# Matmuls of queries with state and scores with values issued one at a time between projection matmuls, instead of in blocks of six

## The reference

```
q, k, v, f_logit: (B=4, H=8, S=768, D=48)
f = sigmoid(f_logit)
for t in range(S):
    state = f[t] * state + k[t] outer v[t]      # 48 x 48 per batch and head
    y[t]  = q[t] @ state
x = y as rows: 3072 tokens x 384
xn = x / rms(x) * rms_g
x  = (silu(xn @ w_gate) * (xn @ w_val)) @ w_out  # d_ff 1536
h  = x @ w_in                                    # d_ff 2048
g  = 0 below -1, h above 1, (h + 1)**2 / 4 between
out = g @ w_out2
```

## Time and profile before

| | |
|---|---|
| median of 3 runs | 1015.99 us |
| span of the profiled execution, first to last instruction | 1013.9 us |
| TensorE matmuls | 1000.9 us busy, 99% |
| TensorE weight loads | 985.1 us busy, 97% |
| DVE | 586.5 us, 58% |
| ACT | 342.7 us, 34% |
| POOL | 19.5 us, 2% |
| mean granted TensorE clock | 0.999 of full speed |
| L334, queries with state | 192 instructions, 278 ns mean |
| L338, scores with values | 384 instructions, 265 ns mean |

### The profile page before, as it was taken

How to read it: one execution, slowest core, us unless ns; L and a number is a source line. 1 busy time by engine, 2 the same in 40 slices (tenths; PEclk the granted TensorE clock), 3 DMA queues, 4 the chain that set the end, 5 groups by cost and what they waited for, 6 DMA issues and landing times.

```text
span 1013.9 us, 16822 instructions
## 1 busy us (share of the span) xinstructions
PE 1000.9 (99%) x6307; PEld 985.1 (97%) x6307; DVE 586.5 (58%) x1196; ACT 342.7 (34%) x624; POOL 19.5 (2%) x58
## 2 busy tenths in 40 slices
PE   7999999999999999999999999999999999999998
PEld 7899999999999999999999999999999999999998
DVE  8777564665565664664663665545554545454553
ACT  2343322322322322222222444344344443434343
POOL 0000000000000000000000000000000000000000
PEclk9999999999999999999999999999999999999999
DMA  5541111111111011111121230000000000000000
GB/s 187 185 143 40 40 39 41 39 39 47 31 46 39 31 47 39 39 39 39 39 68 48 80 92 2 1 23 0 23 0 23 0 23 0 23 0 23 0 24 24
DMA packets 15768, 42.22 MB, mean 42 GB/s; under 512 B 1408, under 2 KB 8064, under 8 KB 15744
## 3 DMA queue, kind: packets, MB, share of 16 engines
q1 hardware_dynamic: 15744, 41.88, 12.3%
HBM read 37.16 MB, written 4.72 MB: 41 GB/s over the span
## 4 chain that ended last, share of the span: by engine, by line
PE 93%; DVE 4%; issue 1%; POOL 1%; ACT 0%; DMA 0%; POOLq 0%; DVEq 0%
PE gate_ps L399 14%; PE val_ps L399 14%; PE acc L475 13%; PE gate_ps L463 10%; PE val_ps L463 10%; PE acc L421 9%; PE acc L479 7%; PE acc L425 5%; PE y_ps L338 4%; PE tb L313 2%; PE y_ps L334 2%; PE tb L322 2%; DVE qd L717 1%; PE ta L299 1%; DVE kd L726 1%
## 5 line engine op out<-in xcount | busy, mean ns | idle before, releaser
L833 DVE TENSOR_TENSOR h_lo<-h_buf,h_hi 128x384 fp32r<-128x384 f32 x224 | 123.2, 550 | 13.2 <-ACT h_hi L644 6.2
L475 PE MATMUL acc<-h_hi,w_hi 128*128 128x384 f32 x381 | 127.5, 335 | 0.0
L475 PE MATMUL acc<-h_hi,w_lo 128*128 128x384 f32 x381 | 127.3, 334 | 0.0
L637 ACT ACTIVATE act_buf<-act_buf,half_col 128x384 f32<-128x384 f32 x128 | 78.7, 615 | 140.4 <-DVE act_buf L883 140.4
L580 ACT ACTIVATE act_buf<-gate_ps 128x384 f32<-128x384 f32 x96 | 47.2, 491 | 180.9 <-PE gate_ps L399 180.9
L399 PE MATMUL gate_ps<-x_hi,w_hi 128*128 (+1 forms) x288 | 100.5, 349 | 2.0 <-DVE h_buf L822 1.5
L585 ACT ACTIVATE h_hi<-h_buf 128x384 fp32r<-128x384 f32 x96 | 50.4, 525 | 151.0 <-DVE h_buf L828 151.0
L421 PE MATMUL acc<-h_hi,w_hi 128*128 128x384 f32 x288 | 100.4, 349 | 0.0
L399 PE MATMUL val_ps<-x_hi,w_hi 128*128 (+1 forms) x288 | 100.2, 348 | 0.0
L399 PE MATMUL gate_ps<-x_hi,w_lo 128*128 (+1 forms) x288 | 96.7, 336 | 0.0
L421 PE MATMUL acc<-h_hi,w_lo 128*128 128x384 f32 x288 | 96.6, 335 | 0.0
(11 more groups left out here) (117 smaller groups left out, 2040.5 us busy)
## 6 DMA issues: line engine op xcount, KB each, us to landing
raw<-qkf_dram SPq DMA_DIRECT2D x21, 768.0 KB, 4.3
x<-wb_dram SPq DMA_DIRECT2D x12, 576.0 KB, 5.9
v_sb<-v_dram SPq DMA_DIRECT2D x24, 192.0 KB, 2.8
out_dram<-x SPq DMA_DIRECT2D x7, 576.0 KB, 2.8
raw<-wc_dram SPq DMA_DIRECT2D x7, 384.0 KB, 3.1
x<-qkf_dram SPq DMA_DIRECT2D x2, 768.0 KB, 6.5
kd<-wc_dram SPq DMA_DIRECT2D x3, 384.0 KB, 3.2
qd<-wc_dram SPq DMA_DIRECT2D x3, 384.0 KB, 3.4
```

The costliest lines, as they stand in the source:

```text
L475: pe.matmul(acc[:, m, 0:N], wc_part(w, j, 1, m), h_hi[:, j % 2, :], start=(j == 0 and w is w_hi), stop=False)
L637: nc.scalar.activation(act_buf[:, j % 2, :], act_buf[:, j % 2, :], ACT.Square, bias=half_col[:, :], scale=0.5).then_inc(square_ready, 1)
L833: nc.vector.tensor_tensor(h_lo[:, j % 2, :], h_buf[:, j % 2, :], h_hi[:, j % 2, :].bitcast(F32), ALU.subtract).then_inc(done, 1)
```

## The change

attend is called with a single step (0 to 5) instead of issuing its six matmuls. A new function, between, issues step m behind the m-th matmul of the nine of the projection group that follows the slot: behind each of the first six matmuls of value 3, project_out 2, project_out 5, gate 7, gate 10 and value 10. The semaphore waits of the block stand at its first step, y_made's increment at its last. turn_kd and turn_x also take an index, but are still called in full at their slots, and first_attention keeps its order. The number of instructions is the same on every engine, and nothing changes on ACT, DVE, POOL and SP.

```diff
...
-                def attend(n, c, half):
-                    if half == 0:
+                def attend(n, c, half, step):
+                    p, part = half * NP // 2 + step // 3, step % 3
+                    o = p * 2 * D
+                    if half == 0 and step == 0:
                         pe.wait_ge(scores_ready, n * 2 + 2)
                         pe.wait_ge(decayed_ready, n + 1)
                         if not isinstance(n, int) or n > 0:
                             pe.wait_ge(xs_ready, n)
-                    for p in range(half * NP // 2, (half + 1) * NP // 2):
-                        o = p * 2 * D
-                        pe.matmul(y_ps[:, o:o + 2 * D], qd[0:PR, c % 2, p, :], decayed[0:PR, p, :],
-                                  start=True, stop=False, skip_group_check=True)
-                        for r in range(2):
-                            h = slice(o + r * D, o + (r + 1) * D)
-                            mm = pe.matmul(y_ps[:, h], scores[:, r, p, :], v_sb[:, r, p, :],
-                                           start=False, stop=True, skip_group_check=True)
-                    mm.then_inc(y_made, 1)
-
...
                         elif o == 8:
                             update(n)
-                        elif o == 9:
-                            attend(n, c, 0)
-                        elif o == 10:
-                            attend(n, c, 1)
                         elif o == 13:
-                            turn_x(n)
+                            for k in range(KM):
+                                turn_x(n, k)
+
+                def between(i, slot, m):
+
+                    if i is None or m > 5:
+                        return
+                    for c in range(CT):
+                        n = i * CT + c
+                        o = slot - WINDOW * c
+                        if o == 9 or o == 10:
+                            attend(n, c, o - 9, m)
 
...
-                def project(i, j, part, bank):
+                def project(i, j, part, bank, following, slot):
 
                     par = i % 2
                     for k in range(KM):
-                        for w, x in ((w_hi, x_hi), (w_hi, x_lo), (w_lo, x_hi)):
+                        for t, (w, x) in enumerate(((w_hi, x_hi), (w_hi, x_lo), (w_lo, x_hi))):
                             mm = pe.matmul(bank[:, 0:N], wb_part(w, j, part, k), x[:, par, k, :],
                                            start=(k == 0 and x is x_hi and w is w_hi),
                                            stop=(k == KM - 1 and w is w_lo))
+                            if k < KM - 1 or t < 2:
+                                between(following, slot, 3 * k + t)
                     return mm
 
-                def gate(i, j):
+                def gate(i, j, following=None, slot=0):
                     pe.wait_ge(w_lo_ready, j + 1)
                     if j == 0:
                         pe.wait_ge(x_lo_ready, i * CT + CT)
                     pe.wait_ge(gate_used, i * JB + j + 1)
-                    project(i, j, 0, gate_ps).then_inc(gate_made, 1)
-
-                def value(i, j):
+                    project(i, j, 0, gate_ps, following, slot).then_inc(gate_made, 1)
+
+                def value(i, j, following, slot):
                     pe.wait_ge(h_ready, i * JB + j + 1)
-                    project(i, j, 1, val_ps).then_inc(val_made, 1)
-
-                def project_out(i, j):
+                    project(i, j, 1, val_ps, following, slot).then_inc(val_made, 1)
+
+                def project_out(i, j, following=None, slot=0):
                     pe.wait_ge(h_hi_ready, i * JB + j + 1)
                     if j == 0:
                         pe.wait_ge(x2_ready, i + 1)
                     for m in range(KM):
-                        for w in (w_hi, w_lo):
+                        for t, w in enumerate((w_hi, w_lo)):
                             pe.matmul(acc[:, m, 0:N], wb_part(w, j, 2, m), h_hi[:, j % 2, :],
                                       start=(j == 0 and w is w_hi), stop=False)
+                            between(following, slot, 2 * m + t)
                     pe.wait_ge(h_lo_ready, i * JB + j + 1)
                     for m in range(KM):
                         mm = pe.matmul(acc[:, m, 0:N], wb_part(w_hi, j, 2, m), h_lo[:, j % 2, :],
                                        start=False, stop=(j == JB - 1))
+                        if m < KM - 1:
+                            between(following, slot, 2 * KM + m)
                     mm.then_inc(out_made, 1)
 
                 def gated_mlp(i, following):
 
                     for j in range(JB):
                         if j > 0:
-                            gate(i, j)
+                            gate(i, j, following, 3 * j - 1)
                         if following is not None:
                             attention(following, 3 * j)
-                        value(i, j)
+                        value(i, j, following, 3 * j)
                         if following is not None:
                             attention(following, 3 * j + 1)
                         if j > 0:
-                            project_out(i, j - 1)
+                            project_out(i, j - 1, following, 3 * j + 1)
                         if following is None and j == 0:
                             pe.wait_ge(least_ready, NCH + 1)
                             pe.transpose(ta[0:1, 0:P], least[:, NP:NP + 1], ident[:, :]).then_inc(least_turned, 1)
```

## The result

The kernel with single steps took 1026.78 us (median of 4 runs, 1026.56 to 1026.95) against 1015.97 for the kernel before: ratio 1.0105, 95% interval 1.0093 to 1.0117. It is 10.8 us slower. The forecast was 1028.2 us.

The account below looks back on a forecast made before the run. TensorE, busy 99% of the span, was taken as the bound. Steps +0.8, late y_made +7.3 in second and +4.1 in first chunks, third 0, sum to +12.2 us over the median of 1015.99: 1028.2 us, range 1016 to 1035.

Parts of the forecast that it names:

- Part 1, the steps themselves: On TensorE, six single steps cost 1.39 us against 1.37 for a block; over 42 blocks +0.8 us.
- 12 bare loads: Lower bound for the steps on TensorE: only 12 loads per block, 1.34 us, giving -1.3 us in all.
- the 0.03 of leftover per block: Block's 1.37 us beyond its 12 loads on TensorE; paid at every step it gave the upper bound, +6.5 us.
- Part 2, second chunk: y_made 1.04 us later passes whole through ACT, POOL and DVE to gate 8's load: 7 x 1.04 = +7.3 us.
- Part 2, first chunk: Late y_made, less slack, delays L425's and gate 5's loads by 0.59 us per tile: +4.1 us.
- Part 2, third chunk: About 0.36 us of the lateness reaches DVE, but turn_x on TensorE reads over 2 us later: 0.
- Rival (a): On TensorE, a step hides one load more than a block: gain 28.2 us, 1000.0 us in total; 12%.
- never sooner: Claim that each TensorE weight load starts with the matmul before it, so loads run exactly one ahead; 1028.2 us.
- The Trainium skill's window of 64: Opposing rule: TensorE pulls weight loads ahead of matmuls in flight; reaching two loads ahead, it would give 1000.0 us.
- Rival (b): Late y_made is absorbed on its way through DVE, leaving only the steps' own cost: 1016 to 1017 us; 8%.
- Rival (c): Changing operand shape or type at each step drains TensorE's array, 0.25 us idle: +53 us on top, 1081 us; 4%.

Follow-up runs that it names:

- after_gate_first: Changed kernel (single steps) with use_gate of steps 4 and 7, and rest_h 3, ahead of the next chunk's decays on DVE: 1012.36 us, ratio 0.9964.
- before_gate_first: Kernel before (blocks of six in their old places) with use_gate likewise ahead of the decays on DVE: 1013.07 us, ratio 0.9974.
- short_loads_block: before_gate_first with attend taking 64 weight columns instead of 128 in tiles 1 to 7: 1003.22 us, ratio 0.9874.
- late_block: Against the kernel before, each block of six kept together but issued behind the sixth big matmul of its group: 1029.11 us, ratio 1.0127.
- second_chunk_only: Kernel before with only the second half of each tile's second chunk issued step by step: 1023.04 us, ratio 1.0068.
- short_loads_steps: after_gate_first with attend taking 64 weight columns instead of 128 in tiles 1 to 7: 1072.59 us, ratio 1.0549.

## Why the prediction was right, by its steps

**Sign, mechanism and size held**: +12.2 forecast, +10.8 measured. Of the 1.4 us between them, half is in the span (1026.1 forecast, 1025.4 measured). The other half is in the 2.1 us that I put around it: they came from the span of one execution and the median of others, while the profiled execution of the changed kernel took 1026.95 us with a span of 1025.4, 1.5 to 1.6 around it.

**Part 1, the steps themselves** (+0.8, bounds -1.3 and +6.5). Six cost 1.34 us and a block 1.34, which makes 0.1 us in 42. after_gate_first and before_gate_first, with nothing waiting, have profiled spans of 1010.5 and 1010.7. So the term is nothing: L443, from which I took 0.01 us per step of extra, was no better a guide than 12 bare loads, and the 0.03 of leftover per block was a matter of where I measured. The step that decides, that loads run one ahead and so 12 of them are exposed either way, is read off the after trace directly. That a pair in a block costs its load is confirmed by short_loads_block, where shorter loads made the pairs cheaper.

**Part 2, second chunk** (+7.3). The wait went from 0.41 to 1.45 us; that step alone gave +7.2 us. Every link passed on 1.03 or 1.04 us; each was already waiting for the one before it.

**Part 2, first chunk** (+4.1). 0.59 forecast per tile, 0.59 in the rows, +4.2 us alone. The slack that was subtracted, 0.45 us, was read as the distance between DVE's end and the load's start, and that was enough.

**Part 2, third chunk** (0). 1.0001. DVE does wait now, 0.28 us ahead of normalise in the after trace, and no reader on TensorE notices.

**The sum.** The two waits make 7 x 1.63 = 11.4 us of the 11.5 by which the profiled spans differ. Of these spans, though, 0.4 us is a later start of the first projection (load at 37.58 instead of 37.17), ahead of any moved step; the 0.3 us that then lack are not the steps, which cost what the blocks cost, and are not traced. I had no term for either; both are below what the times can tell.

**Rival (a)**, a load hidden more, is refuted: a step cost 0.22 us, above its threshold of 0.18. In both traces no load of a projection or of attend starts sooner than the matmul before it. My "never sooner" was too wide all the same: L313 has two matmuls on 64 rows each, and the loads of both start together, 0.10 us before the first of the two matmuls (kernel before, views of loads and of matmuls):

```profile
312.18 0.19 PEld L313 LDWEIGHTS tb<-qd,kd 64*128 64x128 f32 x1
312.18 0.19 PEld L313 LDWEIGHTS ta<-qd,kd 64*128 64x128 f32 x1
...
312.28 0.27 PE L313 MATMUL tb<-qd,kd 64*128 64x128 f32 x1
```

For the projections and attend the reading held. The Trainium skill's window of 64 (TensorE: Matmul & The Clock Gate, "Step-by-step: what each phase is for") did not reach a second load ahead in the steps. **Rival (b)**, an absorbed lateness, is refuted by late_block and second_chunk_only. **Rival (c)** is refuted for the change, whose steps have no idle time ahead of their loads. The idle time itself is there for 64 rows (L313) and for 64 weight columns (short_loads_steps); that it is the array draining is not shown.

What remains open: what in the hardware the idle 0.25 us at such a change of shape is. I saw where it stands, and did not try which shapes cause it.

## What to carry to other kernels

Where the streams of small matmuls are shorter than the next weight load, and the small weights follow the big ones without idle time as they do here with 128 columns, their order is neutral: each load and matmul pair costs one load, alone or in a block. It is not neutral where the change of shape leaves idle time, as with 64 columns (69 us). In the neutral case ask of such a move only when the results come, and follow the reader of the late result through the program order of its engine to what stands behind it; here a product that frees a bank stood behind three engines and 2.5 us of decays. If that chain is already waiting somewhere, cut it there first: setting use_gate ahead of the decays at two steps of a tile gained 3 to 4 us, where moving 252 matmuls lost 11.

## What the runs showed that I had not expected

Some changes of shape between neighbouring weights stop the load from running ahead. With 128 columns beside 128, and 112 rows beside 128 rows, the small load starts 0.17 us after the big one's, hidden. With 64 columns beside 128 it starts 0.37 to 0.44 us after, with 0.18 to 0.25 us of idle time, and the way back costs 0.19 or more instead of 0.11. In blocks only 9 to 10 us of the 25.6 forecast from shorter loads were left; in single steps it cost 69 us more than in blocks.

The 64-row matmuls of L313 had shown the same 0.25 us in the kernel before. Two other shapes in the same trace had not: the lone transpose of L443, one column wide, and the state update L322, whose weights of 112 columns follow the big ones after 0.17 us:

```profile
316.05 0.19 PEld L399 LDWEIGHTS val_ps<-x_hi,w_lo 128*128 128x128 f32 x1
316.22 0.94 PEld L322 LDWEIGHTS tb<-v_sb,kdT 128*112 128x112 f32 x8
```

So a different width is not enough. The idle time stands at 64 columns and at 64 rows, and neither at 112 of either nor at the transpose of one column; what sets them apart is not shown.
